# Attention with four heads on each half of the partitions, second scores with the packs as rows, their turns in 32x32 blocks on VectorE, packing on 64x32 parts

## The reference

```python
def sm_attn(qq, kk, vv):
    s = scale * np.matmul(qq, kk.transpose(0, 1, 3, 2))
    s = s - np.max(s, axis=-1, keepdims=True)
    a = np.exp(s)
    a = a / (np.sum(a, axis=-1, keepdims=True) + 1e-09)
    return np.matmul(a, vv)
p_packed = sm_attn(p, k, v)          # 32 packs look at 576 tokens
out = sm_attn(q, p_packed, p_packed) # 576 tokens look at 32 packs
```

## Time and profile before

| | us |
|---|---|
| median of 3 runs | 1073.85 (1071.5 to 1074.08) |
| the profiled execution | 1072.93 |
| its span, first to last instruction | 1071.0 |
| busy in it: PE / DVE / ACT / POOL | 1051.8 / 609.9 / 372.2 / 235.3 |

### The profile page before, as it was taken

The page is one execution under the profiler, slowest core; times in us unless marked ns, Lnnn a source line. Parts: engine busy times, 40 slices in busy tenths (PEclk is TensorE's granted clock), DMA queues, the critical chain, the costliest instruction groups (busy, mean ns, idle before and its releaser), DMA issues.

```text
span 1071.0 us, 14394 instructions
## 1 busy us (share of the span) xinstructions
PE 1051.8 (98%) x5722; PEld 850.9 (79%) x5722; DVE 609.9 (57%) x1024; ACT 372.2 (35%) x605; POOL 235.3 (22%) x214
## 2 busy tenths in 40 slices
PE   7999999999999999999999999999999999999998
PEld 5676666888888888888888888888888888888887
DVE  3685768776666567765456553656365643663021
ACT  4566765342343243323322142223322241223111
POOL 0111335186794659360000000000000000000000
PEclk9899999999999999999999999999999999999999
DMA  9996772524544346122565435445345535542341
GB/s 257 324 274 211 227 230 82 204 87 172 192 184 160 138 160 238 80 118 108 191 271 199 173 123 200 171 186 196 117 188 207 205 109 187 201 142 90 115 161 40
DMA packets 72371, 185.23 MB, mean 173 GB/s; under 512 B 20848, under 2 KB 45424, under 8 KB 62576
## 3 DMA queue, kind: packets, MB, share of 16 engines
q1 hardware_dynamic: 66080, 149.31, 41.3%
q0 software_dynamic: 6224, 35.00, 8.6%
HBM read 136.71 MB, written 49.68 MB: 174 GB/s over the span
## 4 chain that ended last, share of the span: by engine, by line
PE 86%; DVE 6%; ACT 3%; issue 3%; SPq 1%; DMA 1%; ACTq 0%
PE ps L1168 27%; PE ps L709 25%; PE ps L1200 14%; PE ps L1191 5%; PE ps L884 3%; PE ps L1064 2%; PE ps L718 2%; PE ps L854 2%; PE ps L929 2%; DVE h_lo L1578 1%; DVE spot L1856 1%; DVE spot L1847 1%; DVE bn L1745 1%; PE ps L813 1%; PE ps L908 1%
## 5 line engine op out<-in xcount | busy, mean ns | idle before, releaser
L1168 PE MATMUL ps<-ys,slot 128*128 128x512 f32 x1512 | 346.1, 390 | 0.6
L1168 PEld LDWEIGHTS ps<-ys,slot 128*128 128x128 f32 x1512 | 283.2, 188 | 62.8 <-ACT spot L1243 3.9
L1847 DVE TENSOR_TENSOR spot<-ps,spot 128x512 f32<-128x512 f32 x108 | 74.3, 688 | 103.1 <-PE ps L1168 74.9
L1243 ACT ACTIVATE spot<-ps 128x512 f32<-128x512 f32 x90 | 52.8, 596 | 208.2 <-PE ps L1168 197.1
L709 PE MATMUL ps<-ln_hi,w_out_s_lo 128*128 128x512 f32 x280 | 109.0, 389 | 0.0
L709 PE MATMUL ps<-ln_hi,w_out_s_hi 128*128 128x512 f32 x280 | 108.9, 389 | 0.0
L709 PE MATMUL ps<-ln_lo,w_out_s_hi 128*128 128x512 f32 x280 | 108.9, 389 | 0.0
L1200 PE MATMUL ps<-w_out_s_lo,h_hi 128*128 128x512 f32 x216 | 84.0, 389 | 0.0
L1200 PE MATMUL ps<-w_out_s_hi,h_hi 128*128 128x512 f32 x216 | 84.0, 389 | 0.0
L1200 PE MATMUL ps<-w_out_s_hi,h_lo 128*128 128x512 f32 x216 | 84.0, 389 | 0.0
L1389 ACT ACTIVATE u<-ps,neg_max 128x1024 f32<-128x1024 f32 x36 | 40.2, 1118 | 120.1 <-DVE neg_max L1727 120.1
(11 more groups left out here) (155 smaller groups left out, 1580.0 us busy)
## 6 DMA issues: line engine op xcount, KB each, us to landing
slot<-w_operands SPq DMA_DIRECT2D x36, 1792.0 KB, 7.3
w_operands<-stage POOLq DMA_DIRECT2D x18, 1024.0 KB, 4.7
y_features<-yst SPq DMA_DIRECT2D x9, 1024.0 KB, 4.5
y_raw<-y_features SPq DMA_DIRECT2D x9, 1024.0 KB, 5.4
out_dram<-spot SPq DMA_DIRECT2D x36, 256.0 KB, 2.0
slot<-w_operands SPq DMA_DIRECT2D x9, 1024.0 KB, 5.1
k_raw<-in_k_dram SPq DMA_DIRECT2D x32, 256.0 KB, 6.4
v_raw<-in_v_dram SPq DMA_DIRECT2D x8, 1024.0 KB, 6.2
```

The costliest lines, as they stand in the source:

```text
L1168: last = pe.matmul(ps[:, group_bank(g, k), :], w[:, a - 1, i, kk, :], ys[:, b, j, kk, :], start=n < 4 and kk == 0 and e == 0, stop=kk == K ...
L1243: return act.activation(dst, src, ACT.Copy)
L1847: dve.tensor_tensor(dst[:, :], a, b, op).then_inc(ready, 1)
```

## The change

Heads 0 to 3 now lie on partitions 0 to 63 and heads 4 to 7 on partitions 64 to 127, with nine tokens on each partition. So there is no tail: each load of k, v or q goes to 64 partitions, in runs of 2304 bytes, once for each half. The second scores get the form of the first: rows are packs, four heads on 32 rows each, and tokens are columns (`scores`, used by both). A softmax over packs would then run across partitions, so VectorE turns blocks of 32x32: `turn_in` from PSUM to SBUF, where tokens become rows and packs columns in each block, and `turn_out` back after the softmax. The subtraction of the maximum moves to GpSimd (`sub2`). `turn_a2` and `copy_a2` are gone. `pack` has 72 matmuls with 32 columns of weights and 64 moving columns, each on one of eight 64x32 parts. The merges move ahead of the first scores of the same step, w_out is loaded without the copy through memory, and `split_w_out` stands behind the stores. The two turning banks are taken in turn by a table.

```diff
-            def load_turned(b, view, full, tail, loaded, used=None):
-                for x in range(PAIRS + 1):
-                    if used is not None:
-                        wait_alone(sp, used, TILES * (b - 1) + x + 1)
-                    dst, src = (full[:, 2 * x:2 * x + 2, :, :].rearrange("p h j d -> p h (j d)"),
-                                view[0][b, :, 2 * x:2 * x + 2, :]) if x < PAIRS else \
-                        (tail[0:TAIL, :, :], view[1][b])
-                    sp.dma_start(dst, src).then_inc(loaded[x], 16)
...
+            def load_k(b):
+                if b > 0:
+                    sp.wait_ge(kT_filled, (QH + 1) * b)
+                for x in range(2):
+                    for g in range(QUADS):
+                        sp.dma_start(k_raw[half(g), 2 * x:2 * x + 2, :, :].rearrange("p h j d -> p h (j d)"),
+                                     k_v[b, g][:, 2 * x:2 * x + 2, :]).then_inc(k_loaded[x], 16)
...
+            def load_q(b):
+                if b > 0:
+                    sp.wait_ge(qT_filled, (QH + 1) * b)
+                for g in range(QUADS):
+                    sp.dma_start(q_raw[half(g), :, :, :].rearrange("p h j d -> p h (j d)"), q_v[b, g])\
+                        .then_inc(q_loaded, 16)
...
-                load_k_p(b + 2)
-                load_v_q(b + 1)
-                if b == 0:
-                    sp.dma_start(w_out_dram, w_out_v).then_inc(w_out_moved, 16)
-                if b == 1:
-                    sp.wait_ge(w_out_moved, 16)
-                    sp.dma_start(w_out_raw(0, K1), w_out_dram).then_inc(w_out_loaded, 16)
+                load_k(b + 2)
+                load_p(b + 2)
+                load_v(b + 1)
+                load_q(b + 1)
                 if b == 0:
                     sp.dma_start(w_in_s[:, :, :], w_in_v).then_inc(w_in_loaded, 16)
-            load_v_q(B - 1)
+                if b == 1:
+                    sp.dma_start(w_out_raw[:, :, :], w_out_v).then_inc(w_out_loaded, 16)
...
+            def sub2(b, g):
+                pool.wait_ge(m2_ready, QUADS * b + g + 1)
+                pool.tensor_tensor(quad(g), quad(g), spread(m2, g), ALU.subtract).then_inc(s2_sub, 1)
+            def scale2(b, g):
+                pool.wait_ge(inv2_ready, QUADS * b + g + 1)
+                pool.tensor_tensor(quad(g), quad(g), spread(inv2, g), ALU.mult).then_inc(a2_ready, 1)
...
             for b in range(B - 1):
-                for n in range(S2_PARTS):
-                    scale2(b, n)
-                if b > MEAN_STEP:
-                    split_w_out(b - MEAN_STEP - 1)
+                for g in range(QUADS):
+                    sub2(b, g)
+                for g in range(QUADS):
+                    scale2(b, g)
                 if b >= 2:
                     store_weights(b)
                     store_merged(b)
+                if b > MEAN_STEP:
+                    split_w_out(b - MEAN_STEP - 1)
...
+            def scores(g, out, small, x):
+                for h in range(QH):
+                    rows = slice(h * NPACK, (h + 1) * NPACK)
+                    pe.matmul(out[rows, 0:HALF], small(0, h), ones_cols(x, h, g), start=True, stop=True)
                 for jj in range(2):
                     part = slice(jj * D, (jj + 1) * D)
-                    for h in range(4):
-                        at = (4 * g + h) * 2 * P
-                        last = pe.matmul(out[rows[h], TAIL + jj * 2 * P:TAIL + (jj + 1) * 2 * P], pT[part, g, rows[h]],
...
+                    for h in range(QH):
+                        rows = slice(h * NPACK, (h + 1) * NPACK)
+                        last = pe.matmul(out[rows, HALF + jj * MAIN:HALF + (jj + 1) * MAIN], small(jj, h),
+                                         main_cols(x, part, h, g), start=True, stop=True)
+                return last
...
+            def pack(b):
+                pe.wait_ge(v_loaded, 32 * b + 32)
+                pe.wait_ge(a1T_first, 2 * b + 2)
+                pe.wait_ge(a1T_second, b + 1)
+                for m in range(J):
+                    for h in range(QH):
+                        rows = slice(h * NPACK, (h + 1) * NPACK)
+                        for g in range(QUADS):
+                            last = pe.matmul(ps[rows, u_banks[g], 0:D], a1T[half(g), m, rows],
+                                             v_raw[half(g), h, token_of(m), :], start=m == 0, stop=m == J - 1)
...
-            def scores2(b, n):
...
-                if n == 2:
-                    pe.wait_ge(s2_sub, S2_PARTS * b + 1)
-                if n < 2:
-                    for h in range(H):
-                        last = pe.matmul(bank[:, h * 2 * NPACK:(h + 1) * 2 * NPACK], qT[:, head_cols(h, 2 * n)],
-                                         packedT[b % 2][:, h, :, :], start=True, stop=True)
-                else:
-                    for pair in range(PAIRS):
-                        last = pe.matmul(bank[0:TAIL, pair * 2 * NPACK:(pair + 1) * 2 * NPACK], qT[:, tail_cols(pair)],
-                                         pair_of(packedT[b % 2], pair), start=True, stop=True)
-                last.then_inc(s2_filled, 1)
...
-            def turn_a2(b, n):
-                bank = ps[:, a2T_bank(n), :]
-                wait_alone(pe, a2_ready, S2_PARTS * b + n + 1)
...
-                for jj, j in enumerate(range(2 * n, min(2 * n + 2, TILES))):
-                    w = width(j)
-                    for g in range(QUADS):
-                        at = (1 - jj) * 2 * P + g * w if n < 2 else g * w
-                        last = pe.transpose(bank[:, at:at + w], a2[0:w, j, 4 * g:4 * g + 4, :], ident[0:w, 0:w])
-                last.then_inc(a2T_filled, 1)
...
+            def scores2(b, g):
+                pe.wait_ge(*turn_done("packed", b))
+                pe.wait_ge(*turn_done("q", b, QH - 1))
+                pe.wait_ge(*turn_done("q", b, QH))
+                wait(pe, s2_turned, QUADS * b + g)
+                def small(jj, h):
+                    return packedT[b % 2][jj * D:(jj + 1) * D, QH * g + h, 1 - jj, :]
+                scores(g, scores_cols(mid_banks[0]), small, qT).then_inc(s2_filled, 1)
...
-            def sub2(b, n):
-                dve.wait_ge(s2_filled, S2_PARTS * b + n + 1)
-                src, mx = s2_bank(n, ps[:, mid_banks[n % 2], :]), s2_rows(m2, n)
-                dve.tensor_reduce(mx, src, AX.X, ALU.max).then_inc(m2_ready, 1)
-                dve.wait_ge(m2_ready, S2_PARTS * b + n + 1)
-                dve.tensor_tensor(s2_rows(a2, n), src, mx.unsqueeze(len(mx.shape)).broadcast_to(list(src.shape)),
-                                  ALU.subtract).then_inc(s2_sub, 1)
...
+            def turn_in(b, g):
+                dve.wait_ge(s2_filled, QUADS * b + g + 1)
+                wait(dve, a2T_ready, 3 * b)
+                dve.transpose(a2[:, g, :], scores_cols(mid_banks[0])).then_inc(s2_turned, 1)
+            def quad(g):
+                return a2[:, g, :].rearrange("r (k n) -> r k n", n=NPACK)
+            def max2(b, g):
+                dve.wait_ge(s2_turned, QUADS * b + g + 1)
+                dve.tensor_reduce(m2[:, g, :], quad(g), AX.X, ALU.max).then_inc(m2_ready, 1)
...
+            def turn_out(b, g):
+                if g == 0 and 0 < b < 3:
+                    dve.wait_ge(a_low, b if b < 3 else 2)
+                elif g == 0 and 2 < b < B - 1:
+                    dve.wait_ge(a_stored, 16 * (b - 2))
+                dve.wait_ge(a2_ready, QUADS * b + g + 1)
+                dve.transpose(tokens_main(a2T_of(b), g), a2[:, g, HALF:S]).then_inc(a2T_ready, 1)
+                if g == QUADS - 1:
+                    dve.transpose(tokens_ones(a2T_of(b)), a2[:, :, 0:HALF]).then_inc(a2T_ready, 1)
```

715 lines of the change are left out of this document (309 added, 406 removed).

## The result

The changed kernel takes 1096.4 us (median of 4 runs, 1094.8 to 1097.4) against 1072.7 for the kernel before on the same chip: 1.022 times, 95% interval 1.020 to 1.025. It is 23.7 us slower. The profiled execution took 1094.8 us for a span of 1093.2.

The account below looks back on a forecast made before the run. TensorE was busy 98%; after the change, transfers of 18.8 us would set a steady step, against 20.4 before. Gaining 10.8 us up to step 5's end and 2 in the tail, 12.8 together, gave 1060 us, range 1041 to 1079.

Parts of the forecast that it names:

- Where the gain would be and what the rest keeps: Only the attention stage changes; the 861.8 us from the first `down` on keep their instructions.
- TensorE spared: Steady step: 2.7 us off second scores, 1.2 off turning weights back, 1.4 off packing; TensorE's work falls to 14.8 us.
- The price of a tensor: Loading k, q or v to 64 partitions at a time takes 5.1 us each, between 3.4 and 5.7.
- What the transfers of a step add up to: Steady step: 3 x 5.1 us for tensors, 0.5 for p, 3 to 4.4 for stores: 18.8 us, longer than the engines' chain.
- rival B: Halves load at 5.7 us a tensor with stores in series, 22.0 us a step; kernel 1078.5, up to 1088; chance 0.22.
- The slow clock behind a wait: With 22.0 us steps TensorE stands 5 us, then its clock falls to 1.2 GHz, as an earlier 7 us stretch lost about 3.
- The tail: Step 6 and the last step fall from 49.95 to 48 us: 5 of 7 us spared are lost to late engine work.
- a sign of being wrong: The prediction is wrong if VectorE sets the step, or if the last two steps grow instead of shrinking.
- The chain of 16.2 us: Steady step through the engines, 14.8 us of TensorE work and waits of 1.2 to 1.5, takes about 16.2 us.
- rival A: Halves load as fast as whole tensors, 3.4 us each, so the engines' chain decides; kernel 1040 to 1046; chance 0.29.

Follow-up runs that it names:

- the slim run: The changed kernel with the packing cut to its first and last token block, 16 matmuls in place of 72, result not the reference's: 1093.8 us.
- the last one: The changed kernel, loads still to 64 partitions, with the packing in 36 matmuls and two edits of order for the tail: 1080.3 us.
- tiny loads: The changed kernel with k, q and v transfers from the second batch on cut to 256 bytes per head to one partition: 1068.7 us.
- the wide packing: The changed kernel with the packing in 36 matmuls on 64x64 parts, two heads at a time, in place of 72: 1092.3 us.
- the edits of order: The changed kernel with VectorE's third query copy ahead of the second turn out and the last w_out split behind the last subtractions: 1092.6 us.
- the two mends: The changed kernel with the packing in 36 matmuls (1092.3 us alone) and the tail's two order edits (1092.6 us alone); together 1080.3 us.
- the kernel before with halves: The kernel before with each k, q and v transfer split into one to partitions 0 to 63 and one to 64 to 127: 1083.7 us.
- the run with the stores later: The changed kernel with a batch's two stores held back on GpSimd until the next queries have landed: 1111.3 us.

## Why the prediction was wrong

1060 was forecast, within 1041 to 1079; the time is 36 us above the first and 17 above the second. The first `down` starts 34.4 us later than forecast. By place: 9.0 of it up to the end of step 0, 8.0 in step 1 (25.6 us against 17.6), 3.4, 2.9 and 4.5 in steps 3 to 5, 7.6 in the last two steps, and step 2 is 1.1 shorter. By the steps of the prediction:

- **Where the gain would be and what the rest keeps**: right. Behind the first `down` nothing changed but 1 us.
- **TensorE spared**: nearly right. Score groups take 0.68 us as forecast. The packing takes 1.87 us where it runs through, not 1.4. Step 4 without its waits and the slow clock is 21.7 - 4.2 - 0.6 - 1.5 = 15.4 us, forecast 14.8. The Trainium skill (TensorE: Matmul & The Clock Gate, Back-to-back issue gap) gives 62 ns a matmul where the sequencer decodes it, an estimate of 4.5 us for the packing. The trace has 26 ns for each of the 72 and doesn't bear this out; whether the sequencer decodes them here it doesn't show.
- **The price of a tensor**, 5.1 us: nearly right. Quarters of k land 1.24 us apart, 5.0 us a tensor; the packets of 163 ns in step 4 and 173 ns up to 51.7 us make it 5.2 and 5.5. By the Trainium skill (SBUF — State Buffer, Door 1) half transfers reach half the ports; the runs bear out the direction (1096.4 against 1071.3, and 1083.7 against 1071.9 in the kernel before) with 226 to 230 GB/s instead of its 196.
- **What the transfers of a step add up to, 18.8 us: the step that failed.** It let the stores fill gaps, for 3 us. There is no gap to fill: in step 4 the packets of the loads add up to 15.6 us of all 16 engines, the stores to 4.9, p's 256-byte packets to 0.9 (0.5 was counted), in all 21.9 us with small ones. The step takes 21.7 us, and 22.7 and 22.0 in the slim run and in the last one, which have no stop in it either. This is rival B's sum, 22.0 us, with the tensors cheaper and the rest dearer; B had a chance of 0.22. The same fault stands in the early steps. Up to the landing of w_in at 51.7 us (45.6 was forecast) the packets of the tensors, seven and a part of the next k, take 42.0 us, p's 2.5 and w_in's 6.2, at a DMA share of 1.05. In step 1, forecast as long as the chain, the packets of the loads and of w_out add up to 24.3 us with small ones (the forecast put w_out's time into step 2). Step 5, 23.3 us, is another case: its DMA engines stand at 0.66, and a stop of 4.8 us lies in it. The slow clock behind a wait, named in B, is there (0.78). B's 1078.5 to 1088 fell short for the next two points.
- **Not in the prediction at all: the stops in the packing**, which come at the edges of 256 records and are fewer with fewer matmuls. What they cost depends on what lies behind them: next to nothing while the loads are late (1093.8 with none of them and less work), 5.2 us of their 14.7 where the loads have room (1070.5 to 1065.3).
- **The tail**, forecast 48 against 49.95 before, took 55.1: it grew, which the prediction had called a sign of being wrong. The mechanism was named, `split_w_out` ahead of the last subtraction; its size was not. The subtraction starts at 206.0, `exp2` at 207.2, the second `exp_h` behind it, and TensorE waits 2.0 us for merged_last; and the wait for VectorE's query copy behind the turns out, 3.5 us, was counted as one like the 1.2 to 1.5 of a steady step. Both mended: 50.0.
- **The chain of 16.2 us**: too short. Steps with tiny loads take 18 us. Turns in take 780 ns (760 forecast), turns out, which write tokens nine apart, 1101 (691 forecast):

```profile
L1570 DVE STREAM_TRANSPOSE a2T<-a 128x512 f32<-128x512 f32 x14 | 14.8, 1101 | 0.2
L1542 DVE STREAM_TRANSPOSE a<-ps 128x576 f32<-128x576 f32 x16 | 12.5, 780 | 9.6 <-PE ps L781 9.5
```

So rival A, fast halves at 1040 to 1046, was too good also: with full rates, the wide packing and the edits of order it is 1060.3. That this is the forecast's number is luck: transfers that cost less than it said and a chain that costs more cancel. What is not settled is why the two mends together gave 16 us on halves and 4 each singly. In the profiled execution with the edits of order alone the stops were longer than after (31.9 us against 20.2); whether they would be so each time was not tried. Nor was v tried on all partitions with the result kept: the packing needs each head group on its own half.

## What to carry to other kernels

A layout that puts data on half of the partitions is paid for in each load. Price the transfers of a step as packets in series, stores and one-time loads included, before counting what the engines are spared, and look first at the DMA engines' share: 0.77 of 20.4 us before is 15.7 us of transfers, most of it loads, and at two thirds of the rate they don't fit in 18. When a repaired stall brings nothing, look for the wait that took its place, and repair both before judging either. On a queue that an engine of the chain runs in order, the last item of side work (here a split of weights, a copy) belongs behind the chain's link, not ahead of it.

## What the runs showed of the hardware

- TensorE stands in the middle of long rows of short fp32 matmuls. With a packing of 16 matmuls there was no such stop, with 36 (five kernels) none to three of 0.2 to 2.2 us, with 72 (ten kernels) two to ten of 0.2 to 6.4 us. All 84 of them over 0.15 us, in the profiled executions of these kernels, ended 1.2 to 1.7 us behind the end of a 16 KB packet of the instruction queue, also where hardly any loads ran (8.8 us in all). All 84 stand at the same place of a row of 256 TensorE records, number 193 (449, 705, 961 and so on in the kernel after). That TensorE waits there for the next packet of its instructions is read from this; no record names it. By the rows the packing uses 288 records in 1.87 us, while a packet takes about 1.2 us and is used 1.2 to 1.7 us later. Why an edge is a stop in one batch and not in another was not tried. (An 8.4 us wait put down to "issue" in the kernel before with halves is another thing: it ends with w_in, which landed at 58.44. So are two of 0.2 us in the run with the stores later, which lie elsewhere in the row.)
- A transfer whose source has an outermost dimension of 2 took the time of two of 16 DMA engines (13.0%): 51 GB/s.
- Transfers to 64 partitions: 226 to 230 GB/s, quarters of 288 KB 1.24 us apart; 208 GB/s with the halves from two queues. Stretches with loads to 128 partitions: 312 to 345 GB/s.
- VectorE's turns in 32x32 blocks: 128x576 fp32 from PSUM to SBUF 780 ns, 128x512 within SBUF with the writes nine apart 1101 ns.
- Copies from PSUM that write every fourth column took 1.15 us instead of 0.60 on ScalarE and 1.06 instead of 0.68 on VectorE; matmuls of 256 columns that read columns 2 KB apart 1.07 instead of 0.61 us a group of twelve, and no longer than that with runs of 16 neighbours.
